# Attention scores of the later units as paired fp32 products, with slots, opening transfers and the last sums' banks set anew

## The reference

```python
# attention, for B=2, H=8, S=768, D=40
m_new = max(f + m, i); f_stab = exp(f + m - m_new); i_stab = exp(i - m_new)
C = f_stab * C + i_stab * outer(v, k);  n = f_stab * n + i_stab * k
y = sigmoid(o) * (C @ q) / max(|n . q|, 1)
# experts, for N=1536 tokens, D=320, F=1024, E=4
p = domain_probs / domain_probs.sum(-1)
for e in range(E):
    out += p[:, e] * (relu(x @ w1[e]) @ w2[e])
```

## Time and profile before

| what | value |
|---|---|
| median of 3 runs | 407.63 us |
| lowest and highest | 406.55 and 408.7 us |
| the profiled execution | 409.92 us |
| its span in the profile | 408.0 us |
| mean granted clock of PE | 0.995 |
| PE busy | 402.0 us, 99% |
| DVE, ACT, POOL busy | 263.5, 192.4, 193.7 us |
| moved by the transfers | 54.48 MB |

### The profile page before, as it was taken

The page is one execution under the profiler, slowest core; times in us unless marked ns, Lnnn a source line. Parts: engine busy times, 40 slices in busy tenths (PEclk is TensorE's granted clock), DMA queues, the critical chain, the costliest instruction groups (busy, mean ns, idle before and its releaser), DMA issues.

```text
span 408.0 us, 7284 instructions
## 1 busy us (share of the span) xinstructions
PE 402.0 (99%) x2650; PEld 388.7 (95%) x2650; DVE 263.5 (65%) x490; ACT 192.4 (47%) x378; POOL 193.7 (47%) x227
## 2 busy tenths in 40 slices
PE   8999999999999999999999999999999999999997
PEld 8898999999999999999999999889899989999996
DVE  6873966786465555475259893677666666667653
ACT  5583647845264478444116433353454345434420
POOL 5854843476053889832502001568435553556300
PEclk9998999999999999999999999999999999999999
DMA  7889909878263585261025002222112211230002
GB/s 275 278 280 382 372 35 292 328 260 277 96 227 104 181 258 199 82 212 48 2 49 123 0 2 84 86 72 98 31 54 84 85 42 43 84 102 17 0 2 96
DMA packets 18052, 54.48 MB, mean 134 GB/s; under 512 B 2177, under 2 KB 8850, under 8 KB 16866
## 3 DMA queue, kind: packets, MB, share of 16 engines
q1 hardware_dynamic: 17442, 52.63, 38.0%
q10 hardware_dynamic: 576, 1.40, 1.0%
HBM read 50.40 MB, written 2.05 MB: 129 GB/s over the span
## 4 chain that ended last, share of the span: by engine, by line
PE 92%; DMA 3%; DVE 1%; SPq 1%; POOL 1%; issue 0%; ACT 0%; DVEq 0%
PE acc_ps L1641 21%; PE hid_ps L1622 21%; PE acc_ps L1707 15%; PE out_ps L1578 4%; PE hid_ps L1707 3%; DMA w_raw<-in_w_b 3%; PE out_ps L1683 2%; PE out_ps L1684 2%; PE out_ps L1686 2%; PE out_ps L1685 2%; PE acc_ps L1622 2%; PE score_ps L1522 2%; PE out_ps L1585 2%; PE add_ps L1683 1%; PE add_ps L1684 1%; PE score_ps L1684 1%
## 5 line engine op out<-in xcount | busy, mean ns | idle before, releaser
L1165 DVE SCALAR_TENSOR_TENSOR h_lo<-hid_ps,h_hi 128x384 fp32r<-128x384 f32 (+1 forms) x72 | 36.8, 512 | 79.5 <-ACT h_hi L821 79.2
L821 ACT ACTIVATE h_hi<-hid_ps 128x384 fp32r<-128x384 f32 (+1 forms) x72 | 32.8, 455 | 106.2 <-PE hid_ps L1622 106.0
L1641 PE MATMUL acc_ps<-w_hi,h_hi 128*128 128x320 f32 x208 | 66.3, 319 | 0.0
L1641 PE MATMUL acc_ps<-w_hi,h_lo 128*128 128x320 f32 x208 | 64.2, 309 | 0.0
L1641 PE MATMUL acc_ps<-w_lo,h_hi 128*128 128x320 f32 x208 | 64.0, 308 | 0.0
L1622 PE MATMUL hid_ps<-xt_hi,w_hi 128*128 128x384 f32 (+1 forms) x216 | 58.0, 323 | 0.1
L1622 PE MATMUL hid_ps<-xt_hi,w_lo 128*128 128x384 f32 (+1 forms) x216 | 57.6, 320 | 0.4 <-POOL w_lo L624 0.4
L624 POOL TENSOR_TENSOR w_lo<-w_raw,w_hi 128x384 fp32r<-128x384 f32 x40 | 43.4, 1088 | 19.1 <-ACT w_hi L807 19.1
L694 POOL TENSOR_TENSOR w_hi<-w_raw,w_hi 128x640 fp32r<-128x640 f32 x12 | 19.5, 1623 | 51.7 <-ACT w_hi L864 51.7
L1641 PEld LDWEIGHTS acc_ps<-w_hi,h_hi 128*128 128x128 f32 x208 | 39.4, 189 | 0.2
L598 POOL TENSOR_SCALAR_AFFINE_SELECT dec_w<-dec_w 128x512 f32<-128x512 f32 x22 | 14.9, 678 | 51.8 <-ACT dec_w L786 51.8
(11 more groups left out here) (251 smaller groups left out, 994.0 us busy)
## 6 DMA issues: line engine op xcount, KB each, us to landing
w_raw<-in_w_b SPq DMA_DIRECT2D x19, 704.0 KB, 7.3
w_raw<-in_w_s SPq DMA_DIRECT2D x12, 832.0 KB, 4.6
raw<-in_qk_s SPq DMA_DIRECT2D x8, 1024.0 KB
g_all<-g_dram SPq DMA_DIRECT2D x10, 512.0 KB, 6.2
kv<-in_kv_n SPq DMA_DIRECT2D x12, 352.0 KB, 6.0
q_pack<-in_q_p SPq DMA_DIRECT2D x10, 192.0 KB, 6.4
out_y<-y_acc SPq DMA_DIRECT2D x12, 160.0 KB, 1.8
carry<-g_dram SPq DMA_DIRECT2D x30, 60.0 KB
```

Source lines behind the costliest of these rows:

```text
L821: nc.scalar.activation(h_hi[:, M % RING, 0:cols], hid_bank(M)[:, 0:cols], ACT.Relu).then_inc(hid_hi, 1)
L1165: nc.vector.scalar_tensor_tensor(h_lo[:, M % RING, 0:cols], hid_bank(M)[:, 0:cols], 0.0, h_hi[:, M % RING, 0:cols].bitcast(fp32), ALU.max, ...
L1641: last = nc.tensor.matmul(acc_ps[t][:, 0:DM], x, w, start=(f == 0 and i == 0), stop=(f == NF - 1 and i == 2))
```

## The change

**Scores.** Units 2 to 11 now work as units 0 and 1 did. The array `qk_p` holds heads 0 to 3 in rows 0 to 39 and heads 4 to 7 in rows 64 to 103, so that a transfer is 512 KB (1024 KB before for units 4 to 11, 416 KB for units 2 and 3). `scores(k)` issues eight fp32 products, alternately into `score_ps` and `add_ps`, in slot `T0[k]`. The cast, the subtraction, the zeros and their semaphores go. Since `add_ps` also takes the sums of `additions`, `scores(k)` waits until `keep_heads` of the unit before has read it (`fresh_ready`), `additions(k)` waits for both `probs` of its unit, and `keep_heads` moves ahead of `gate_x`, one slot earlier.

**Slots and transfers.** `T0`, `OPEN_IN` and `LATER_PAIRS` get other numbers, and `reload_scores` another place. Blocks 16 to 27 of the down-projection's low parts go from DVE to POOL. `carry_state` follows `split_low` within a slot. In SP's opening, pairs 3, 4 and 5 of the weights stand further ahead.

**The last sums.** In steps 10 and 11 the second half's sums go to `hid_ps`, `score_ps` and `out_ps` instead of the three `acc_ps`, and they are issued ahead of the first half's.

```diff
-T0 = {2: 2, 3: 6, 4: 16, 5: 20, 6: 26, 7: 32, 8: 36, 9: 48, 10: 52, 11: 56}
+T0 = {2: 2, 3: 7, 4: 14, 5: 21, 6: 26, 7: 31, 8: 36, 9: 44, 10: 49, 11: 56}
-DN_FIRST, DN_END = 0, 28
-OPEN_IN = {3: (2,), 13: (4,), 14: (6,), 17: (8,), 18: (10,)}
-LATER_PAIRS = {12: 8, 14: 9, 16: 10}
+DN_FIRST, DN_END = (0, 16)
+OPEN_IN = {5: (2,), 9: (4,), 12: (6,), 16: (8,), 18: (10,)}
+LATER_PAIRS = {12: 8, 16: 9, 18: 10}
+AGAIN = 2
+LAGS = {'carry': 6, 'probs': 2, 'scale': 2}
+        late_acc = [hid_ps[0], score_ps, out_ps]
+        def sum_bank(half, p, i):
+            return late_acc[i] if half == 1 and p >= STEPS - 2 else wide_acc[i]
...
             load_g(2)
+            load_pair(sp, 3)
             sp.wait_ge(out_done, 1)
             sp.wait_ge(add_done, 1)
             load_kv(sp, 2)
             load_carry(2)
-            load_pair(sp, 3)
+            load_pair(sp, 4)
             load_g(3)
             reload_scores(3)
+            load_pair(sp, 5)
             sp.wait_ge(out_done, 2)
             sp.wait_ge(add_done, 2)
             load_kv(sp, 3)
             load_carry(3)
-            load_pair(sp, 4)
-            load_pair(sp, 5)
             load_pair(sp, 6)
             load_pair(sp, 7)
-            reload_scores(4)
...
-                if M == T0[3] + 4:
-                    reload_scores(5)
-                if (k := unit_at(M, -2)) is not None and NS <= k < NT - 2:
+                if (k := unit_at(M, AGAIN)) is not None and k + 2 < NT:
                     reload_scores(k + 2)
...
-                for k, t in taken_in(CAST, M):
-                    cast(k, t)
...
                 if (k := unit_at(M, 4)) is not None:
+                    if k < NT - B:
+                        keep_heads(k)
                     gate_x(k)
...
-                for k, t in taken_in(SUB, M):
-                    subtract_high(k, t)
-                if (k := unit_at(M, 5)) is not None and k < NT - B:
-                    keep_heads(k)
...
+            def scores(k):
+                pe.wait_ge(qk_in[kept(k)], scores_in(k))
+                pe.wait_ge(p_ready, 2 * k)
+                pe.wait_ge(fresh_ready, min(k, NT - B))
+                for a in range(HALF):
+                    for half, bank in ((0, score_ps), (1, add_ps)):
+                        rows = slice(64 * half, 64 * half + D)
+                        product = nc.tensor.matmul(bank[:, a * L:(a + 1) * L], raw[rows, kept(k), 1, a, :],
+                                                   raw[rows, kept(k), 0, a, :], start=True, stop=True)
+                        if a == HALF - 1:
+                            product.then_inc(s_ready, 1)
...
-                    pe.wait_ge(fresh_ready, max(k, 1))
+                    pe.wait_ge(fresh_ready, k)
+                    pe.wait_ge(p_ready, 2 * k + 2)
...
+                    elif half == 1 and p == STEPS - 2:
+                        if i == 0:
+                            pe.wait_ge(acc_free, LATE_FREED)
+                        else:
+                            pe.wait_ge(low_of[(0, 11, 21)[i]], STEPS)
...
-                ahead, behind = halves_of(t)
+                ahead, behind = halves_of(t) if t != STEPS else halves_of(t)[::-1]
```

More of the change, by code:

```diff
@@ L180, in bank_freed @@
     return wide_evictions(p - 2, 1, min(i, pairs(p - 2) - 1))
+LATE_FREED = max(wide_evictions(p, 1, PAIRS - 1) for p in range(1, STEPS, 2) if pairs(p) == PAIRS)
 def order_of(t):
@@ L277, in build @@
         x_nat = first("x_nat", [L, B, DM])
-        apart = raw[:, :, :, :, :].rearrange("p k t h l -> p k (t h l)")
         attention.close()
@@ L416, in load_scores @@
                 return
[L417 to L421, removed]
+            eng.dma_start(raw[:, kept(k), :, :, :].rearrange("p t h l -> p (t h l)"), qk_p[k - B]).then_inc(qk_in[kept(k)], 16)
         def scores_in(k):
-            return 16 * (k // 2 + 1)
+            return 16 * (k // 2)
         def load_kv(eng, k):
@@ L727, in _ @@
                         weigh_keys(k)
-                if (k := unit_at(M, 2)) is not None:
+                if (k := unit_at(M, LAGS['scale'])) is not None:
                     scale_q(k)
-                if (k := unit_at(M, 6)) is not None and k < NT - B:
-                    carry_state(k)
                 for w in blocks_to_split(M):
                     split_low(w)
+                if (k := unit_at(M, LAGS['carry'])) is not None and k < NT - B:
+                    carry_state(k)
                 if M in (59, 61):
@@ L1095, in probs @@
                 nc.vector.tensor_tensor(prob[:, kept(k), half, :, :].rearrange("p h l -> p (h l)"),
-                                        score_bank.get((k, half), score_ps)[:, :],
+                                        score_bank.get((k, half), (score_ps, add_ps)[half])[:, :],
                                         dec(k, half).rearrange("p h l -> p (h l)"), ALU.mult)\
                     .then_inc(p_ready, 1)
-            def subtract_high(k, t):
-                rows = (slice(64, 64 + D), slice(0, D))[t]
-                dve.wait_ge(cast_done, 2 * (k - NS) + t + 1)
-                hi = split_qk[rows, kept(k), t, :, :]
-                nc.vector.tensor_tensor(hi, raw[rows, kept(k), t, :, :], hi.bitcast(fp32), ALU.subtract)\
-                    .then_inc(sub_done, 1)
             def gate_x(k):
@@ L1706, in wide_down @@
                     for j, (x, w) in enumerate(((hi, w_1), (hi, w_2), (lo, w_1))):
-                        last = nc.tensor.matmul(wide_acc[i][:, 0:DM], x, w, start=(p % 2 == 0 and f == 0 and j == 0),
+                        last = nc.tensor.matmul(sum_bank(half, p, i)[:, 0:DM], x, w, start=(p % 2 == 0 and f == 0 and j == 0),
                                                 stop=(p % 2 == 1 and f == 1 and j == 2))
@@ L1743, in _ @@
                 if (k := unit_at(M, 0)) is not None:
-                    scores(k, 0)
-                if (k := unit_at(M, 2)) is not None:
-                    scores(k, 1)
+                    scores(k)
                 if (k := unit_at(M, 6)) is not None:
@@ L1801 @@
         first[:, 64 * odd:64 * odd + D, 0], first[:, 64 * odd:64 * odd + D, 1] = q[:B, :, odd::2], k[:B, :, odd::2]
+    paired = _np.zeros((NT - B, 128, 2, HALF, L), q.dtype)
+    for half in range(2):
+        rows, heads = slice(64 * half, 64 * half + D), slice(half * HALF, (half + 1) * HALF)
+        paired[:, rows, 0], paired[:, rows, 1] = q[B:, :, heads], k[B:, :, heads]
     steps = _np.zeros((len(EXPERTS), NF // 2, 128, SUM_AT), q.dtype)
```

66 lines of the change are left out of this document (9 added, 57 removed).

## The result

The changed kernel takes 409.7 us (409.24 to 409.84, 4 runs), against 407.6 (406.55 to 408.7, 4 runs) before. The ratio is 1.0042, interval [1.0023, 1.0061]. A second measurement, of 10 runs beside 22 of the kernel before, gave 409.72 against 408.20, ratio 1.0033 [1.0018, 1.0048]. The change makes this kernel slower by 0.3 to 0.4%, where a gain of 0.6% was forecast; 409.7 lies outside the range.

The account below looks back on a forecast made before the run. Bound: PE's work, plus 3.49 us lost in the opening and 0.32 near the end. Sum: -0.49 - 1.19 - 1.71 + 0.3 + 1.0 - 0.32 = -2.4 us, giving 405.2 from the median; range 403.0 to 408.2.

Parts of the forecast that it names:

- The last step: Whole kernel: the profiled execution's forecast drop, 409.92 to 407.5, was also taken off the median 407.63, giving 405.2.
- a fall of the clock: Opening, 38.65 to 42.06 us: PE's clock at its lower level, 1.71 us lost, taken as gone; bounds 0 and 1.71.
- the two stalls: Up-projections at 29 and 37 us, late weight low parts: 0.59 and 1.19 us lost, forecast to save 0.49 and 1.19.
- Rival (a): Opening: the clock still falls once; 406.9 us, chance 0.14.
- PE's work for scores: Scores of units 2 to 11: ten paired units at 1.15 us, 11.5 against 10.5 before, +1.0 us; bounds -1.2 and +4.2.
- small waits in slots 6 to 10: After the opening, PE running ahead of ACT and POOL: 0.3 us charged, bounds 0 and 1.0.
- Rival (b): Scores, changes of array tiling: full drains, 1.47 us a unit, 408.4 us; half of it, 1.31, gives 406.8; chance 0.14.
- The opening: SP's early transfers: pair 4 lands 4.5 us sooner, at 32.4; both stalls (all but 0.1 us) and the clock's fall go.
- ACT, POOL, the added waits: Work moved off DVE and ACT, low parts given to POOL, scores waiting for `keep_heads`: each taken as 0 us.
- (c): Slots 20 to 25: POOL is late, 1.5 us more, 406.7 us; chance 0.07.
- (d): Scores of units 3, 6, 7, 8 and 10: PE waits for `add_ps`; at 1.0 us each, 410.2 us; chance 0.06.
- The end: Second half's sums of step 10 no longer wait for DVE's evictions: -0.32 us.

Follow-up runs that it names:

- the run again: The kernel before, run again with no edit: 408.1 us, ratio 0.9998.
- the run with the last sums: The kernel before with only the last sums' banks and their order changed: 407.74 us, ratio 0.9985.
- the two-piece kernel: The changed kernel with the opening order of before and `raw` of units 2 and 3 brought in two transfers: 413.35 us, ratio 1.0119.

## Why the prediction was wrong

In one execution, 409.92 was to become 407.5; the profiled one after took 409.24. From that to the forecast of the median there was one more step. Two steps failed: this one, and the price of a paired unit.

**The last step, "I take the same difference off the median".** This is the larger error. The sum of -2.4 holds 1.71 us for a fall of the clock. The profiled execution had paid for one; its own 2.29 us above the median were the hint, and the prediction even said that they are "about what one fall of the clock costs". Then it took the 1.71 off a median of runs that have none: 97 of 105 show full clock. That also the two stalls vary (0.2 to 1.2 us in two traces at full clock) goes the same way. The profiled execution after stands 0.46 below its median, not 2.29 above: 2.7 us of the 4.5 by which the forecast missed. The 407.63 was besides a median of three runs, 0.6 under the usual 408.2. Rival (a) had named the case in its last sentence ("The median before may also hold runs without a fall, with the same effect"), at 0.14.

**PE's work for scores, the term "1.15 a unit".** The mechanism was right, the size was not: 1.28 to 1.29 measured, by the starts and by two experiments. Missing were 0.04 of the entry (0.10 for 0.06) and 0.10 that falls only on the second whole-array product behind the pairs. Unit 0 could not show that one, since what follows it there are two short products of 16 rows. Ten units at 0.14 more are 1.4 us of the 1.7 by which the profiled execution missed. The unit taken away was put at 0.88 and costs 0.89.

**Terms at nothing.** The slots of the units were moved and DVE's order with them, and the sum had no term for it. The two delays behind DVE, 0.5 us together, stand there; the prediction counted a wait of PE for DVE between 40 and 100 us among the signs of being wrong. Against them, the 0.3 us charged for small waits in slots 6 to 10 did not come. So units 4 to 11 cost 3.9 us, where the sum had 8 x 0.27 = 2.2 for them: 1.1 more for the paired units, 0.5 for the delays, and 0.2 not placed.

**Rival (b)** had this in it: its half-way case of 1.31 us is nearly what was measured. Its prices of 408.4 and 406.8 were too low mainly because they stood on the same median step. The rule of the Trainium skill (TensorEngine Tiling (Array Packing), "Key Properties") that spoke against the change is borne out in kind: with twice as many changes each added one, in and out, cost 0.39 us. It gives no duration. A full wait for a product's 0.27 us was not seen; the longest step is 0.10 over its kind.

**Units 2 and 3** save what was said: by slot 13 the sum said -0.49 - 1.19 - 1.71 + 0.3 and 2 x (1.15 - 1.72) = -4.2, and the traces show -4.05. The match is partly luck: the two units saved 0.86 and not 1.14, the small waits of 0.3 did not come, and 0.18 of the lead was there before unit 2 began (24.09 against 23.91 at the up-projection for slot 4).

**The opening.** That both stalls go, and the fall with them, was right, and pair 4, started near 22 us, was 7.1 us under way. The working was not: it gave the gain to the new order of SP, 1.46 MB that pair 4 no longer waits for. The order alone left stalls in the kernel before, and with the old order the changed kernel had none. What brought them back there was `raw` of units 2 and 3 in two pieces. The prediction had no term for that: it priced the four transfers by their bytes, 416 KB among them, and the bytes rise to 512 KB while the queue gets through sooner. In the first expectation on the old order I had even written that they are halved, which is wrong.

**ACT, POOL, the added waits.** At 0, as said: no delay of PE behind 14 us is put down to `fresh`, to POOL's `w_lo` or to the scaled q, so (c) and (d) did not come. **The end**: -0.41 for -0.32.

**What would have been right.** From a usual run of before, 408.2: units 2 and 3 save 0.86 (from 4 x 0.86 to 2 x 1.29), the end 0.4, and units 4 to 11 cost 3.9. The stalls are best read from starts too, since the list of waits shows only part of them. From the up-projection for slot 4 to that for slot 13 the kernel before took 28.87 us in the run again and 28.03 in the run with the last sums, the changed kernel 26.4 to 26.6; less the 0.86, the stalls are 0.6 to 1.6 us. Together 409.2 to 410.2, and 409.7 was measured.

## What to carry to other kernels

Before a saving is taken off a median, ask whether the median has paid for what is saved: a profiled execution 2 us above it, with a low clock in one slice, is no usual run. Price a change of the array's tiling by the steps on both sides of it, up to the second product behind, and among the neighbours that it will have; then spend it only where it replaces something dearer (1.29 for 1.72 us a unit here, and not for 0.89). A list of waits does not show every delay; the distances of starts, slot by slot against the same slot before, do. And when a transfer changes its form, look at the GB/s of its stretch and not at its bytes alone.

## What the runs showed of the hardware

- Going from products on the whole array to pairs on row halves and back costs 0.39 us here, in four steps of about 0.10 each (the experiments with twice as many changes and with twice the products): before and after the first pair, after the last, and after the first whole-array product.
- Two fp32 products of 40 rows on the two halves start together every 0.11 us, in alternation. In blocks of four products a half they still overlap at the seam, by three records (0.55 us more a unit). Eight fp32r products on the whole array, doubled, cost 0.89 us, the same.
- A transfer of 64 and one of 40 partitions in place of one of 128 lowered the opening's rate from 380 to 257 GB/s (28 to 32 us) and from 407 to 259 (32 to 36) at the same DMA share, with fewer bytes (one trace of each, on two chips). Why, the traces don't show; whether it is the 40, the 64 or the number of transfers wasn't tried apart.
- Behind stalls of PE of 1.2 and 0.3 us at 38 to 40 us the granted clock was at its lower level (0.50) from 40 to 44 us, in the profiled run of the two-piece kernel; 5 of its 6 runs have a low mean clock. In the kernel before, whose opening stalls are smaller, it fell in 8 of 105, and in the kernels with `raw` in one piece in none of 74.
